# One-hot products of the routing in bf16, two of them on GpSimd, and a gate exponential issued earlier

## The chip, the cores and the metric

The kernel runs on one core of one Trainium2 chip. The metric is the device time of one execution in microseconds. A core has a matrix engine (TensorE, PE in the profile; PEld is its weight load), a vector engine (VectorE, DVE), an activation engine (ScalarE, ACT), GpSimd (POOL) and a queue that issues most DMAs (SyncE, SP). The engines run side by side and wait for each other only through semaphores; each engine takes its own instructions in order.

## The reference

Three parts follow one another: attention over 4 x 8 heads of 576 tokens, a gated feed-forward with a spatial mix, and a mixture of 8 experts. The change is in the routing of the third part. In short:

```python
logits = einsum('bsd,de->bse', x, w_gate)              # 4 x 576 tokens, 8 experts
local_gate = 1 / (1 + exp(-(x @ w_local)))
for b, s in tokens:                                    # in order within a batch row
    fresh = argmax(logits[b, s])
    e = fresh if s == 0 or local_gate[b, s] < 0.5 else prev_e
    p = softmax(logits[b, s])
    out[b, s] = p[e] * (relu(x[b, s] @ w1[e]) @ w2[e])
```

So every token gets one expert, which may be the one of the token before it, and a weight p[e].

## The kernel before

The kernel is written engine by engine, with the order of each engine set by hand and with semaphores between them; no planner is at work. Tokens lie as 128 partitions by F = 20 columns (5 tiles of 128 rows by 4 batch rows, the last tile partly filled). After the last feed-forward group the routing works out, for each token, a position in a list sorted by expert. The list is cut into NSLOT = 25 tiles of 128 rows, each tile of one expert. A token's position is then a tile number (`tile_of`) and a row number (`row_of`).

The table `slots` (128 rows by 25 tiles by 2 numbers: the token number and the weight) is made by products on TensorE. VectorE makes `tile_hot` (L1274: 1 where the column is the token's tile, 20 x 25 numbers on each partition), `entries` (L1277 and L1279: `tile_hot` times the token number, kept as the number less 2304 in `token_less`, and `tile_hot` times `weight`) and `row_hot` (L1283: 1 where the column is the token's row, in five parts of 4 x 128 numbers). All are f32. As each part of `row_hot` is ready, TensorE takes 4 products `row_hot` x `entries` (L1343) into one bank, 20 products in all, each adding 50 columns. VectorE reads the sums out of the bank into `slots` (L1295 and L1296).

The helper `step` is what sets the pace of VectorE here: it gives an instruction an increment of the semaphore `routed`, and lets VectorE wait for that same increment before it goes on. `mark` keeps the count under a name for other engines to wait for.

The order on VectorE around this stretch is: last small steps on positions, `tile_hot`, `weight` (L1276, without a wait of its own), two `entries`, five parts of `row_hot`, three copies of the steering numbers (L1287, L1290), then `low_parts(dve, (0, 0, 1), "w1")`, which makes the low halves of the first expert's w1 in four pieces (L1120), and only then the wait for `slots_summed` and the two copies into `slots`. After that come the low halves of w2, again four pieces. Each piece of L1120 waits for its high half, a cast of ScalarE (L1476), and that waits until the expert's weights have landed.

When `slots` is there, GpSimd copies the token numbers of a tile (L1396) and gathers the 128 token rows by an indirect DMA (L1399). TensorE turns them (L1596), ScalarE and VectorE split them into a high and a low part (L1481, L1536), and the expert products begin (L1611 to L1613). From there TensorE runs through all tiles to the end.

Ahead of the routing, in the last group of tokens, ScalarE copies five turned tiles of x2 from the two places of `tbank` to SBUF (L912); each is stored to DRAM by SP, in two DMAs (L864 after the fourth tile, L867 after the fifth), and SP's loads of the expert weights (L1358, L1360) wait until both stores have landed. TensorE may turn tile m only when tile m-2 has been copied (a wait on `x2_out`). The logits are turned after the second tile and taken to SBUF by VectorE (L996). After its five copies ScalarE loads another activation table and takes the two exponentials, of the gate (L1303) and of the logits less their maximum (L1305), and VectorE waits for both ahead of L1215.

Of the kernel before, what the change touches and what calls it, by code (L numbers as in the profile page):

```python
# [5 lines left out]
ALU = mybir.AluOpType  # L6
ACT = mybir.ActivationFunctionType
# [10 lines left out]
def moe_block(nc, q, k, v, s, w_in, g_ln, w_sg, b_sg, w_out, w_gate, w_local, w1, w2, out):  # L18
# [34 lines left out]
    with stack:  # L53
# [31 lines left out]
        iota_p = sb("iota_p", [P, P], F32)  # L85
        token_less = sb("token_less", [P, ST, B], F32)
# [109 lines left out]
        tile_of = eb("tile_of", [P, F], F32)  # L196
        row_of = eb("row_of", [P, F], F32)
        tile_hot = eb("tile_hot", [P, F, NSLOT], F32)
        entries = eb("entries", [P, F, 2, NSLOT], F32)
        row_hot = eb("row_hot", [P, F, P], F32)  # L200
# [98 lines left out]
        slots_summed = sem("slots_summed")  # L299
        expert_in = [sem(f"expert_in{e}") for e in range(E)]  # L300
# [535 lines left out]
        CONSTS = 6 + 9  # L836
# [37 lines left out]
        def _(act):  # L874
# [27 lines left out]
            def tokens_out(b):  # L902

                for n in range(2):
                    act.wait_ge(logits_mm, 2 * b + n + 1)
                    nc.scalar.copy(logT[:, halves[n]], obank[0:E + 1, n, 0:HALF]).then_inc(logT_done, 1)
                act.wait_ge(x2_stored, 16 * (FROM + 2 * b))
                stand_alone(act)
                for m in range(ST):
                    r = rows_of[m]  # L910
                    act.wait_ge(x2_turned, ST * b + m + 1)
                    nc.scalar.copy(x2[0:r, m, :], tbank[0:r, m % 2, :]).then_inc(x2_out, 1)  # L912

# [10 lines left out]
            tokens_out(B - 1)  # L924
# [212 lines left out]
        def _(pool):  # L1137
# [41 lines left out]
            nc.gpsimd.iota(token_less[:, :, :], pattern=[[P, ST], [S, B]], base=-TOK, channel_multiplier=1,  # L1179
# [3 lines left out]
        def _(dve):  # L1183
# [87 lines left out]
            def over_tokens(x, n):  # L1271
# [3 lines left out]
                                         over_tokens(iota_t[:, :], NSLOT), ALU.is_equal))  # L1275
            nc.vector.tensor_reduce(weight[:, :, :], weigh[:, :, :, :], AX_X, ALU.add)  # L1276
            step(nc.vector.tensor_tensor(entries[:, :, 0, :], tile_hot[:, :, :],  # L1277
                                         over_columns(token_less[:, :, :].rearrange("p t b -> p (t b)"), NSLOT), ALU.mult))
            step(nc.vector.tensor_tensor(entries[:, :, 1, :], tile_hot[:, :, :],  # L1279
                                         over_columns(weight[:, :, :].rearrange("p t b -> p (t b)"), NSLOT), ALU.mult))  # L1280
# [14 lines left out]
            step(nc.vector.tensor_scalar(slots[:, :, 0].bitcast(I32), obank[:, 1, 0:NSLOT], float(TOK), None, ALU.add))  # L1295
            step(nc.vector.tensor_copy(slots[:, :, 1], obank[:, 1, NSLOT:2 * NSLOT]))  # L1296
            mark("slots_done")

        @block.scalar
        def _(act):  # L1300
            lg = logit[:, :, :, :].rearrange("p b t e -> p (b t) e")
            act.wait_ge(logits_left, FROM + B)
            nc.scalar.activation(rgate[:, :], lg[:, :, E], ACT.Exp, scale=-1.0).then_inc(route_exp, 1)  # L1303
            act.wait_ge(routed, 2)
            nc.scalar.activation(rexp[:, :, :], rdiff[:, :, :], ACT.Exp).then_inc(route_exp, 1)  # L1305

        @block.tensor
        def _(pe):
# [31 lines left out]
            for n in range(ST):  # L1340
                pe.wait_ge(routed, marks[f"rows_done{n}"])
                for f in range(n * B, (n + 1) * B):
                    mm = nc.tensor.matmul(obank[:, 1, 0:2 * NSLOT], row_hot[:, f, :],  # L1343
                                          entries[:, f, :, :].rearrange("p a n -> p (a n)"),
                                          start=(f == 0), stop=(f == F - 1))
# [39 lines left out]
        def _(pool):  # L1385
            pool.wait_ge(x2_stored, 16 * (FROM + 2 * B))
            pool.wait_ge(zero_stored, 16)
            pool.wait_ge(routed, marks["slots_done"])
# [344 lines left out]
```

## Time and profile before

| | us |
|---|---|
| median of 3 runs | 942.02 |
| lowest and highest | 939.26, 942.26 |
| span of the profiled execution | 940.1 |
| PE busy in it | 873.8 (93%) |
| DVE busy | 517.7 (55%) |
| ACT busy | 405.3 (43%) |
| POOL busy | 99.3 (11%) |

The profile is of one execution. Its page gives busy times, the chain of work that ended last, and the costliest groups of instructions; the timeline gives single instructions with their start, and the idle time of the engine before them with what ended it. L12 is line 12 of the kernel. The granted clock of TensorE is 1.00 at 2.4 GHz and 0.50 at 1.2 GHz.

### The profile page before, as it was taken

Reading aid. Unit: us, or ns where it says so; the run is one execution under the profiler, and the core shown is the slowest. Engines: PE = TensorE matmul, PEld = TensorE weight load, DVE = VectorE, ACT = ScalarE, POOL = GpSimd, SP = SyncE. Lnnn points to the kernel's source line nnn. Section 1 sums busy time; section 2 is a strip of 40 time slices with the busy share of each in tenths; the row PEclk is TensorE's granted clock in tenths of the full one; section 3 lists DMA queues with packets and bytes.
Section 4 is the critical chain, followed back from the end, with each engine's and each line's share of the span. In section 5 each row is a group of like instructions: output and inputs, shape, how many; then the busy total and the mean of one; then the engine's idle time right before and its main releaser. Section 6 shows DMA issues by size and latency. Waiting matters only on the chain.

```text
span 940.1 us, 19053 instructions
## 1 busy us (share of the span) xinstructions
PE 873.8 (93%) x5573; PEld 725.9 (77%) x5574; DVE 517.7 (55%) x1021; ACT 405.3 (43%) x990; POOL 99.3 (11%) x187
## 2 busy tenths in 40 slices
PE   4899999999999989999999999748999999999993
PEld 2677778787787769988988989546888888888773
DVE  6567767777677743624535335384556266536221
ACT  2566666666666644215134142233435244415110
POOL 0001111111111020000000000001111111111111
PEclk9999999999999989999999999858999999999997
DMA  6422232222323100001001001196345255511100
GB/s 165 146 66 66 58 70 53 67 62 58 71 52 71 39 20 1 1 1 50 0 0 50 0 0 52 57 351 224 117 147 201 77 199 205 210 49 35 38 33 21
DMA packets 100842, 74.88 MB, mean 80 GB/s; under 512 B 81416, under 2 KB 81416, under 8 KB 100778
## 3 DMA queue, kind: packets, MB, share of 16 engines
q1 hardware_dynamic: 96810, 63.21, 22.1%
q0 software_dynamic: 4000, 11.28, 3.7%
q8 instruction: 16, 0.26, 0.1%
q14 instruction: 16, 0.13, 0.0%
HBM read 64.43 MB, written 11.86 MB: 81 GB/s over the span
## 4 chain that ended last, share of the span: by engine, by line
PE 90%; DVE 3%; DMA 2%; SPq 2%; issue 2%; ACT 1%; POOL 0%; POOLq 0%; ACTq 0%; DVEq 0%
PE sbank L1020 24%; PE obank L728 10%; PE sbank L1611 9%; PE sbank L1613 9%; PE sbank L1612 9%; PE tbank L709 5%; PE sbank L694 5%; PE sbank L696 3%; PE obank L719 2%; PE tbank L672 2%; PE obank L1068 2%; PE tbank L677 1%; PE tbank L1596 1%; PE tbank L1636 1%; PE sbank L701 1%
## 5 line engine op out<-in xcount | busy, mean ns | idle before, releaser
L455 ACT ACTIVATE probs<-sbank,nmax 128x128 f32<-128x128 f32 (+4 forms) x160 | 90.8, 568 | 55.3 <-DVE nmax L585 55.2
L728 PE MATMUL obank<-pT,v_raw 128*64 128x128 f32 (+2 forms) x960 | 113.2, 262 | 0.3 <-ACT recipT L474 0.3
L728 PEld LDWEIGHTS obank<-pT,v_raw 128*64 128x64 f32 (+1 forms) x960 | 91.5, 136 | 11.4 <-ACT recipT L474 0.5
L585 DVE TENSOR_REDUCE nmax<-sbank 128x1 f32<-128x128 f32 (+4 forms) x160 | 86.5, 541 | 15.4 <-PE sbank L701 12.0
L694 PE MATMUL sbank<-k,q 128*128 128x256 f32 (+2 forms) x192 | 76.6, 404 | 0.8 <-ACT probs L455 0.8
L1611 PE MATMUL sbank<-w_high,xsT_h 128*128 x184 | 74.8, 407 | 2.0 <-DVE xsT_l L1536 1.7
L1120 DVE TENSOR_TENSOR w_low<-w_low,w_high (+1 forms) x64 | 74.0, 1216 | 0.7 <-ACT w_high L1476 0.3
L709 PE MATMUL tbank<-ident,probs 128*128 128x128 f32 (+2 forms) x480 | 73.9, 267 | 0.2 <-ACT probs L455 0.2
L1613 PE MATMUL sbank<-w_low,xsT_h 128*128 x184 | 72.6, 395 | 0.0
L1612 PE MATMUL sbank<-w_high,xsT_l 128*128 x184 | 72.4, 394 | 0.0
L1611 PE MATMUL sbank<-w_high,hidT_h 128*128 x176 | 70.9, 403 | 0.2
L1476 ACT CAST w_high<-w_low (+1 forms) x64 | 62.3, 1052 | 17.4 <-SPq L1365 17.4
L1613 PE MATMUL sbank<-w_low,hidT_h 128*128 x176 | 68.8, 391 | 0.0
L1612 PE MATMUL sbank<-w_high,hidT_l 128*128 x176 | 68.6, 390 | 0.0
L696 PE MATMUL sbank<-k,q 128*128 128x256 f32 (+2 forms) x192 | 60.8, 321 | 0.0
L709 PEld LDWEIGHTS tbank<-ident,probs 128*128 128x128 f32 (+2 forms) x480 | 47.6, 139 | 8.3 <-issue 5.6
L1499 ACT CAST hidT_h<-tbank 128x512 fp32r<-128x512 f32 x22 | 12.9, 586 | 92.3 <-PE tbank L1636 92.3
L1572 DVE TENSOR_SCALAR y<-sbank,sid 128x512 f32<-128x512 f32 x22 | 16.5, 750 | 63.6 <-PE sbank L1613 62.7
L591 DVE COPY pT<-tbank 128x256 f32<-128x256 f32 x64 | 35.7, 558 | 26.1 <-PE tbank L709 26.1
L562 DVE TENSOR_TENSOR k<-tbank,k 64x512 fp32r<-64x512 f32 x64 | 28.7, 449 | 38.5 <-ACT q L450 38.2
L1020 PE MATMUL sbank<-wsg_h,vn_h 128*128 128x288 f32 x160 | 47.5, 297 | 2.2 <-DVE vn_l L954 1.9
L1407 POOL DMA_INDIRECT out_dram<-y,sid x25 | 25.3, 1010 | 217.2 <-DVE y L1572 214.1
(230 smaller groups left out, 1983.5 us busy)
## 6 DMA issues: line engine op xcount, KB each, us to landing
w_low<-in_moe_w_dram SPq DMA_DIRECT2D x16, 2048.0 KB, 13.4
k_raw<-in_k_dram SPq DMA_DIRECT2D x64, 128.0 KB, 2.3
q_raw<-in_q_dram SPq DMA_DIRECT2D x32, 128.0 KB, 2.3
v_raw<-in_v_dram SPq DMA_DIRECT2D x32, 128.0 KB, 2.2
x_dram<-x SPq DMA_DIRECT2D x4, 1024.0 KB, 4.4
win_raw<-in_moe_w_in_dram SPq DMA_DIRECT2D x1, 2048.0 KB, 8.0
wsg_raw<-in_moe_w_sg_dram SPq DMA_DIRECT2D x1, 1152.0 KB, 6.3
k_raw<-in_k_dram SPq DMA_DIRECT2D x64, 16.0 KB, 2.1
```

The lines of the kernel that those rows point to most:

```text
L455: nc.scalar.activation(probs_view(u, i, r), score_view(i, r), ACT.Exp, bias=nmax[u][0:r, i:i + 1], accum_out=sums[u][0:r, i:i + 1]).then_i ...
L585: nc.vector.tensor_reduce(nmax[u][0:r, i:i + 1], src, ax, ALU.max, negate=True).then_inc(maxed, 1)
L694: nc.tensor.matmul(dst, q1[u][:, q_cols], k1[u][:, cols], start=True, stop=False)
L696: nc.tensor.matmul(dst, q2[u][:, q_cols], k2[u][:, cols], start=False, stop=last)
L709: mm = nc.tensor.transpose(tbank[0:c, 1 if i == 3 else 0, r * j:r * (j + 1)], probs[u][0:r, OFF_P[i] + P * j:OFF_P[i] + P * j + c], ident[ ...
L728: mm = nc.tensor.matmul(obank[0:D, c, a:a + w], v_raw[u][0:r, j, :], pT[0:r, j, P * i:P * i + w], start=(j == 0), stop=(j == i))
L1020: mm = nc.tensor.matmul(dst, a[:, i, lhs_cols], b[:, i, rhs_cols], start=(n == 0), stop=(n == 3 * len(pairs) - 1))
L1120: nc.vector.tensor_sub(w, w.bitcast(F32), piece(w_high, high_place, i).bitcast(F32)).then_inc(wlow_done, 1)
L1476: nc.scalar.copy(piece(w_high, high_place, i), piece(w_low, low_place, i).bitcast(F32)).then_inc(whigh_done, 1)
L1611: nc.tensor.matmul(dst, xh, wh, start=first, stop=False)
L1612: nc.tensor.matmul(dst, xl, wh, start=False, stop=False)
L1613: return nc.tensor.matmul(dst, xh, wl, start=False, stop=last)
```

## The change

The numbers of the one-hot products become bf16. So that nothing is lost, the token number is split in two parts that bf16 holds exactly (a multiple of 64 in `token_high`, 0 to 127 in `token_low`), and the weight in three (`weight_parts`), each being the bf16 rounding of what is left. `entries` so has 5 parts of 25 columns in place of 2. The two of the token number are made by GpSimd, the three of the weight by VectorE. The sums of the parts are taken after the products. The exponential of the gate, with the table load ahead of it, is issued between the second and the third copy of the last group.

```diff
-        iota_p = sb("iota_p", [P, P], F32)
-        token_less = sb("token_less", [P, ST, B], F32)
+        iota_p = sb("iota_p", [P, P], BF16)
+        slot_ids = sb("slot_ids", [P, NSLOT], F32)
+        iota_tb = sb("iota_tb", [P, NSLOT], BF16)
+        token_low = sb("token_low", [P, ST, B], BF16)
+        token_high = sb("token_high", [P, ST, B], BF16)
...
-        tile_of = eb("tile_of", [P, F], F32)
-        row_of = eb("row_of", [P, F], F32)
-        tile_hot = eb("tile_hot", [P, F, NSLOT], F32)
-        entries = eb("entries", [P, F, 2, NSLOT], F32)
-        row_hot = eb("row_hot", [P, F, P], F32)
+        tile_of = eb("tile_of", [P, F], BF16)
+        row_of = eb("row_of", [P, F], BF16)
+        tile_hot = eb("tile_hot", [P, F, NSLOT], BF16)
+        entries = eb("entries", [P, F, 5, NSLOT], BF16)
+        row_hot = eb("row_hot", [P, F, P], BF16)
+        weight_parts = [eb(f"weight_part{n}", [P, ST, B], BF16) for n in range(3)]
+        weight_left = [eb(f"weight_left{n}", [P, ST, B], F32) for n in range(2)]
...
+            def gate_exps():
+                act.wait_ge(logits_left, FROM + B)
+                nc.scalar.activation(rgate[:, :], logit[:, :, :, E].rearrange("p b t -> p (b t)"), ACT.Exp,
+                                     scale=-1.0).then_inc(route_exp, 1)
...
                     nc.scalar.copy(x2[0:r, m, :], tbank[0:r, m % 2, :]).then_inc(x2_out, 1)
+                    if last and m == 1:
+                        gate_exps()
...
             step(nc.vector.tensor_tensor(tile_hot[:, :, :], over_columns(tile_of[:, :], NSLOT),
-                                         over_tokens(iota_t[:, :], NSLOT), ALU.is_equal))
-            nc.vector.tensor_reduce(weight[:, :, :], weigh[:, :, :, :], AX_X, ALU.add)
-            step(nc.vector.tensor_tensor(entries[:, :, 0, :], tile_hot[:, :, :],
-                                         over_columns(token_less[:, :, :].rearrange("p t b -> p (t b)"), NSLOT), ALU.mult))
-            step(nc.vector.tensor_tensor(entries[:, :, 1, :], tile_hot[:, :, :],
-                                         over_columns(weight[:, :, :].rearrange("p t b -> p (t b)"), NSLOT), ALU.mult))
+                                         over_tokens(iota_tb[:, :], NSLOT), ALU.is_equal))
+            mark("tiles_hot")
+            step(nc.vector.tensor_reduce(weight[:, :, :], weigh[:, :, :, :], AX_X, ALU.add))
+            step(nc.vector.tensor_copy(weight_parts[0][:, :, :], weight[:, :, :]))
+            step(nc.vector.tensor_tensor(weight_left[0][:, :, :], weight[:, :, :], weight_parts[0][:, :, :],
+                                         ALU.subtract))
+            step(nc.vector.tensor_copy(weight_parts[1][:, :, :], weight_left[0][:, :, :]))
+            step(nc.vector.tensor_tensor(weight_left[1][:, :, :], weight_left[0][:, :, :],
+                                         weight_parts[1][:, :, :], ALU.subtract))
+            step(nc.vector.tensor_copy(weight_parts[2][:, :, :], weight_left[1][:, :, :]))
+            for n in range(3):
+                step(nc.vector.tensor_tensor(entries[:, :, 2 + n, :], tile_hot[:, :, :],
+                                             over_columns(weight_parts[n][:, :, :].rearrange("p t b -> p (t b)"),
+                                                          NSLOT), ALU.mult))
...
-            step(nc.vector.tensor_scalar(slots[:, :, 0].bitcast(I32), obank[:, 1, 0:NSLOT], float(TOK), None, ALU.add))
-            step(nc.vector.tensor_copy(slots[:, :, 1], obank[:, 1, NSLOT:2 * NSLOT]))
+            parts = obank[:, 1, 0:5 * NSLOT].rearrange("p (a n) -> p n a", n=NSLOT)
+            step(nc.vector.tensor_reduce(slot_ids[:, :], parts[:, :, 0:2], AX_X, ALU.add))
+            step(nc.vector.tensor_scalar(slots[:, :, 0].bitcast(I32), slot_ids[:, :], float(TOK), None, ALU.add))
+            step(nc.vector.tensor_reduce(slots[:, :, 1], parts[:, :, 2:5], AX_X, ALU.add))
...
-                    mm = nc.tensor.matmul(obank[:, 1, 0:2 * NSLOT], row_hot[:, f, :],
+                    if f == 0:
+                        pe.wait_ge(tokens_in, 2)
+                    mm = nc.tensor.matmul(obank[:, 1, 0:5 * NSLOT], row_hot[:, f, :],
...
             pool.wait_ge(zero_stored, 16)
+            pool.wait_ge(routed, marks["tiles_hot"])
+            for n, t in enumerate((token_high, token_low)):
+                x = t[:, :, :].rearrange("p t b -> p (t b)").rearrange("p (f o) -> p f o", o=1)
+                nc.gpsimd.tensor_tensor(entries[:, :, n, :], tile_hot[:, :, :],
+                                        x.broadcast_to([P, F, NSLOT]), ALU.mult).then_inc(tokens_in, 1)
```

Left out above: three small `iota` instructions of GpSimd in place of one, among its constants, and the two lines that took the gate's exponential at its old place.

## Rows read from the trace of the kernel before

**Rows 1.** The page, part 4: the chain that ended last, by engine.

```profile
PE 90%; DVE 3%; DMA 2%; SPq 2%; issue 2%; ACT 1%; POOL 0%; POOLq 0%; ACTq 0%; DVEq 0%
```

**Rows 2.** Windows: from:to, length, PE, PEld, DVE, ACT, POOL busy, clock, DMA, GB/s.

```profile
628.00:631.00 3.00, 3.00 (x15) 2.89 (x14) 2.53 (x3) 2.56 (x3) 0.00 (x0) 0.50 1.05 388
...
639.00:640.00 1.00, 0.74 (x2) 0.65 (x3) 0.01 (x1) 0.00 (x0) 0.74 (x1) 0.50 0.00 0
...
643.00:644.00 1.00, 1.00 (x5) 0.79 (x4) 0.00 (x0) 0.00 (x0) 0.00 (x0) 0.82 1.04 426
```

**Rows 3.** Timeline, one-hot stretch: start, length, engine, line, tiles, shapes, count [idle before].

```profile
619.18 0.67 DVE L1274 TENSOR_TENSOR tile_hot<-tile_of,iota_t 128x500 f32<-128x500 f32 x1
619.89 0.32 DVE L1276 TENSOR_REDUCE weight<-weigh 128x20 f32<-128x160 f32 x1
620.12 0.67 DVE L1277 TENSOR_TENSOR entries<-tile_hot,token_less 128x500 f32<-128x500 f32 x1
620.83 0.68 DVE L1279 TENSOR_TENSOR entries<-tile_hot,weight 128x500 f32<-128x500 f32 x1
...
622.29 8.77 PE L1343 MATMUL obank<-entries,row_hot 128*128 128x50 f32 x40 [4.07 <-DVE row_hot L1283]
...
625.90 4.63 DVE L1120 TENSOR_TENSOR w_low<-w_low,w_high 128x1024 fp32r<-128x1024 f32 x4
631.09 0.18 DVE L1295 TENSOR_SCALAR slots<-obank 128x25 int32<-128x25 f32 x1 [0.56 <-PE obank L1343]
631.31 0.18 DVE L1296 COPY slots<-obank 128x25 f32<-128x25 f32 x1
...
631.74 4.63 DVE L1120 TENSOR_TENSOR w_low<-w_low,w_high 128x1024 fp32r<-128x1024 f32 x4 [0.24 <-DVE slots L1296]
```

**Rows 4.** Timeline, the last token copies, the exponentials and the first steps behind them.

```profile
601.23 0.20 DVE L996 COPY logit<-obank 128x45 f32<-128x45 f32 x1 [5.57 <-PE obank L1087]
...
602.54 0.60 PE L1077 MATMUL tbank<-ident,x2T 128*64 128x128 f32 x4 [0.33 <-ACT x L912]
...
603.18 0.58 ACT L912 COPY x<-tbank 64x512 f32<-64x512 f32 x1 [0.29 <-PE tbank L1077]
603.77 1.28 ACT L1303 ACT_TABLE_LOAD   x1
...
605.21 0.32 ACT L1305 ACTIVATE rexp<-rdiff 128x160 f32<-128x160 f32 x1
605.63 0.18 DVE L1215 TENSOR_SCALAR rgate<-rgate 128x20 f32<-128x20 f32 x1 [2.14 <-ACT rexp L1305]
605.85 0.28 DVE L1216 RECIPROCAL rkeep<-rgate 128x20 f32<-128x20 f32 x1
```

**Rows 5.** Timeline, SP's first weight load and ScalarE's casts of the weights.

```profile
608.97 0.40 SPq L1358 DMA_DIRECT2D w_low<-in_moe_w_dram  x1
...
622.89 7.67 ACT L1476 CAST w_high<-w_low 128x1024 fp32r<-128x1024 f32 x8 [17.36 <-SPq L1365]
```

**Rows 6.** Groups by line and shape, 598 to 640 us: busy us, mean ns, idle before.

```profile
L1283 DVE TENSOR_TENSOR row_hot<-row_of,iota_p 128x512 f32<-128x512 f32 x5 | 3.5, 691 | 0.2
...
L1206 DVE TENSOR_TENSOR rdiff<-logit,rmax 128x160 f32<-128x160 f32 x1 | 0.3, 324 | 0.0
...
L1207 DVE TENSOR_SCALAR requal<-rdiff 128x160 f32<-128x160 f32 x1 | 0.2, 243 | 0.0
```

**Rows 7.** POOL: two groups by line and shape of the whole span, then single instructions.

```profile
L427 POOL CAST q<-q 64x576 fp32r<-64x576 f32 x32 | 21.1, 661 | 175.2 <-ACT q L450 175.2
L432 POOL COPY recip_wide<-recip 128x320 f32<-128x320 f32 x32 | 14.4, 449 | 124.4 <-DVE recip L605 124.4
...
631.67 0.19 POOL L1396 COPY gid<-slots 128x1 int32<-128x1 int32 x1 [285.49 <-DVE slots L1296]
...
634.02 1.27 POOL L1396 COPY gid<-slots 128x1 int32<-128x1 int32 x1
```

**Rows 8.** Timeline, 636 to 640 us: where TensorE starts again.

```profile
636.49 1.12 PE L1596 MATMUL tbank<-ident,xs 128*128 128x128 f32 x4 [5.43 <-DMA xs<-x_dram,gid]
...
639.26 0.79 PE L1611 MATMUL sbank<-w_high,xsT_h 128*128 x1 [1.66 <-DVE xsT_l L1536]
```

More of the change, by code:

```diff
@@ L299, in moe_block @@
         slots_summed = sem("slots_summed")
+        tokens_in = sem("tokens_in")
         expert_in = [sem(f"expert_in{e}") for e in range(E)]
@@ L831, in _ @@
             slot(HEADS + 1, 1, this=False, before=False, after=False)
-        CONSTS = 6 + 9
+        CONSTS = 6 + 11
         MIX, PROJ, VEE, YOU = 0, 2 * KT, 4 * KT, 4 * KT + ST
@@ L900, in gated_high, with tokens_out @@
                     nc.scalar.copy(g_h[:, n % KT, halves[n // KT]], uT[:, n % KT, halves[n // KT]]).then_inc(gh_done, 1)
-            def tokens_out(b):
+            def gate_exps():
+                act.wait_ge(logits_left, FROM + B)
+                nc.scalar.activation(rgate[:, :], logit[:, :, :, E].rearrange("p b t -> p (b t)"), ACT.Exp,
+                                     scale=-1.0).then_inc(route_exp, 1)
+            def tokens_out(b, last=False):
                 for n in range(2):
@@ L923, in _ @@
             gated_high(B - 1)
-            tokens_out(B - 1)
+            tokens_out(B - 1, last=True)
         @block.vector
@@ L1178, in _ @@
                            allow_small_or_imprecise_dtypes=True).then_inc(route_const, 1)
-            nc.gpsimd.iota(token_less[:, :, :], pattern=[[P, ST], [S, B]], base=-TOK, channel_multiplier=1,
+            nc.gpsimd.iota(iota_tb[:, :], pattern=[[1, NSLOT]], base=0, channel_multiplier=0,
+                           allow_small_or_imprecise_dtypes=True).then_inc(route_const, 1)
+            nc.gpsimd.iota(token_high[:, :, :], pattern=[[P, ST], [S, B]], base=-TOK, channel_multiplier=0,
+                           allow_small_or_imprecise_dtypes=True).then_inc(route_const, 1)
+            nc.gpsimd.iota(token_low[:, :, :], pattern=[[0, ST], [0, B]], base=0, channel_multiplier=1,
                            allow_small_or_imprecise_dtypes=True).then_inc(route_const, 1)
@@ L1301, in _ @@
             lg = logit[:, :, :, :].rearrange("p b t e -> p (b t) e")
-            act.wait_ge(logits_left, FROM + B)
-            nc.scalar.activation(rgate[:, :], lg[:, :, E], ACT.Exp, scale=-1.0).then_inc(route_exp, 1)
             act.wait_ge(routed, 2)
```

## The prediction

> **What bounds the kernel now.** I read the page's chain first: TensorE holds 90% of it and VectorE 3% [rows 1]. The routing is the place where that is not so. The windows show the granted clock at 0.50 while TensorE takes the one-hot products and still at 0.50 when it starts again at 639.26; only at 643 does it rise [rows 2, 8]. Behind it TensorE runs tile after tile, so what moves the end is the moment at which `slots` is complete: 631.49 us (631.31 + 0.18) [rows 3]. GpSimd waits for it and starts 0.18 us later [rows 7]; the gather, turning and splitting lead to the first expert product at 639.26 [rows 8]. I take that stretch as rigid: what `slots` gains or loses, the end gains or loses.
>
> Next I read the timeline to see which engine makes `slots` late. Two chains meet in it. TensorE's 40 records of L1343 run from 622.29 to 631.06. VectorE meanwhile has done the one-hot work, the steering copies and four pieces of w1's low half, 625.90 to 630.53, and waits 0.56 us for TensorE at L1295 [rows 3]. This is the most important number here: VectorE's own line is only 0.56 us shorter than TensorE's. The pieces of w1 stand ahead of the wait in the program. Whatever is saved on TensorE beyond 0.56 us is not seen.
>
> **TensorE's products.** 40 records become 20, since bf16 needs one pass where f32 shows two records for each product. At 8.77/40 = 0.22 us each that is 4.4 us; the columns rise from 50 to 125, so the bounds are 4.4 and, were nothing saved, 8.77. The first part of `row_hot` is ready at 622.23 + 3.2 = 625.4 by the sum below, and VectorE asks for the sums at 633.8: at the upper bound TensorE would be 0.4 late; at the lower, which I take because the record count halves for certain, the products follow `row_hot` part by part and end over 4 us before VectorE asks. Gain: the 0.56 us, no more.
>
> **VectorE's line, step by step.**
> - The sum over `weigh` now has a wait: 0.32 + 0.04 in place of the 0.23 from 619.89 to 620.12: +0.13 [rows 3].
> - Five small steps, three roundings and two subtractions on 20 numbers, each with a wait: one such step is 605.63 to 605.85, 0.22 us [rows 4]; 5 x 0.22 = +1.10.
> - `entries` for the weight: three products in place of two for both; GpSimd has the others. One takes 0.71 from start to start [rows 3]: +0.71.
> - The nine large instructions (tile_hot, three entries, five row_hot) in bf16: no 2-byte VectorE instruction is in the trace. Bounds: unchanged (0.67 and 0.69), or half the time per element. The time per element is (669 - 324)/(500 - 160) = 1.01 ns for two inputs; half of it saves 0.25 on each of four and 0.26 on each of five, 2.3 in all. An instruction with one input does show a faster rate at the same size (243 against 324 ns for 160 numbers) [rows 3, 6]. I take unchanged: every large two-input row has 1.0 ns per element, and the repeated operand does not get denser by being narrower.
> - The sums out of the bank: before 0.40 (631.09 to 631.49). After: a reduction of 50 numbers, a scalar step, a reduction of 75. From 0.32 for 160 at 1.01 ns less per number, 0.21 and 0.24; with two waits of 0.04 and the 0.18, 0.71: +0.31 [rows 3, 6].
>
> The unchanged rate has a rule of the Trainium skill behind it, which speaks against this change: the page Vector Engine (DVE) Microarchitecture Reference, section 5.1, says that a two-input instruction takes two 16-bit elements per cycle only if the innermost step of every operand is 1 or -1, and that one element read again and again as an operand ran at one per cycle. Here each of the nine has such an operand. No run here shows it yet; by it the 2.3 us stay unsaved.
>
> **The gate's exponential.** Today the last copy ends at 603.76, then come the table load of 1.28, the gate and `rexp`, which ends at 605.53; VectorE has waited 2.14 for it [rows 4]. Moved, the table load begins once the logits are in SBUF (601.43), ends near 602.75, and the gate near 603.0. The third and fourth copies follow, each 0.54, to 604.1. The fifth tile can only be turned when the third copy is done (603.55) and takes 0.60, so its copy runs 604.2 to 604.8 [rows 4], and `rexp` ends at about 605.12. Gain 0.41. Bounds: 0, and 0.64, the two waits of ScalarE that the load can fill. The price: the two stores of x2, and SP's queue of weight loads behind them, move by the delay of the fourth and fifth copies, about 1.0 us. The load issued at 608.97 goes out near 609.9, and the casts begin at 623.9 in place of 622.89 [rows 5]. VectorE wants the first cast, done at 624.9, at 627.4 or later (625.90 + 1.5) [rows 3]; it is covered by 2.5 us, and by 0.2 even if the 2.3 us above were saved. Without that cover it would cost up to 1.0.
>
> **GpSimd beside VectorE.** The trace has no two-input GpSimd instruction. One input costs (661 - 449)/(576 - 320) = 0.83 ns a number and 0.18 fixed, so 500 numbers are 0.60 us; read one input after the other, 1.01 [rows 7]. TensorE's new wait `tokens_in` is harmless: even at 1.01 each both are done before 622.5, ahead of the first part of `row_hot`. What matters is a row that looks small: GpSimd's copy at 634.02 takes 1.27 us where the same copy took 0.19, and it lies across VectorE's two-input pieces of w1, 1.16 each from 631.74, ending as the third of them ends [rows 3, 7]. So one of the two was kept out of SBUF while the other's instruction ran. The reverse, VectorE kept waiting by GpSimd, is not in the trace. Bounds: 0, and 2 x 1.01 = 2.02. I take an exclusive turn for both, as that row shows. GpSimd starts 0.18 after tile_hot, at 620.03, to 621.04; VectorE's sum has one input and passes, its first rounding would start at 620.25 and waits 0.79; the second product holds the subtraction or the rounding 0.9 more: +1.7, behind which all of VectorE's line is queued, the w1 pieces and `slots` with it.
>
> The rule of the Trainium skill beside it (SBUF — State Buffer, Who interferes with whom) is that VectorE instructions with two SBUF inputs, or in a two-port mode, and GpSimd instructions that read SBUF exclude each other for a whole instruction, whichever began first. The row at 634.02 agrees in one direction. GPSIMD Engine Reference, section 3.1, prices a two-input instruction at 4497 ns for 2048 numbers; an estimate from it is 1.2 us for 500, by which the sum would be about 0.4 us larger.
>
> **The sum.** VectorE's arrival at `slots`: 0.13 + 1.10 + 0.71 - 0.41 + 1.7 = +3.23. Less the 0.56 it no longer waits, with 0.04 between instructions, plus 0.31: `slots` is 3.0 us later, 634.5. Against the profiled execution that is a span of 940.1 + 3.0 = 943.1. The median of the runs is 1.9 above that span, and the shift is carried over to it: 942.02 + 3.0 = 945.0.
>
> **The rivals.**
> 1. No exclusion, rate unchanged. The same sum without 1.7: +1.3, 943.3. For it: the trace shows only GpSimd waiting, so VectorE may have the right of way. Against: an instruction of GpSimd already under way can hardly be stopped.
> 2. Faster, the other side: the nine instructions run at half the time per element, -2.3, and VectorE is not held. Sum 1.3 - 2.3 = -1.0, 941.0. It decides from the point where the nine save more than 1.3 us together, 0.15 each. For it: narrower numbers, and the faster one-input row [rows 6]. Against: the repeated operand. With the exclusion as well it gives +0.7, 942.7.
> 3. GpSimd's products take twice as long, 2.0 us each, for a reason the rows don't show, and hold VectorE throughout: 2 us more, 947.0. `tokens_in` itself would decide only from about 5 us each.
> 4. The change does little, since its target was TensorE's 8.77 us: that is part of each case, the 0.56.
>
> TensorE's clock adds a spread to all: it rose 4.0 us after the restart at 639.26 [rows 2, 8]; each us of that more or less is 0.5 us of products at 1.2 in place of 2.4 GHz. The three runs before span 939.26 to 942.26.
>
> **How the numbers follow.** Forecast 0.55 (945.0, own range 943.8 to 946.5); rival 1 0.23; rival 2 0.14, half of it with the exclusion; rival 3 0.08. The range from 941.5 to 947.0 leaves the faster half of rival 2 and the upper tail outside. A measurement of this kernel tells 0.3% from no change, 2.8 us. Slower by more: two thirds of the forecast and nearly all of rival 3, 0.43. Within: the other third, rivals 1 and 2, 0.53. Faster: 0.04, only rival 2 with a kind clock.
>
> **What would show it.** In the new profile: the nine instructions at 0.67 to 0.69 us (or 0.4: rival 2); a VectorE step of 20 numbers near 620.3 that takes 0.8 to 1 us in place of 0.18 (or none: rival 1); GpSimd's two rows at 1.0 us; no wait at the first read of the bank; L1343's successor with 20 records, done 4 us before VectorE comes; the table load at 601.5. The prediction is wrong if `slots` is not later, or if the stretch from `slots` to 639.26 is not rigid.

## The result and the profile after

| | before | after |
|---|---|---|
| median of 9 runs, us | 941.17 | 944.42 |
| lowest and highest | 939.26, 942.26 | 942.43, 946.05 |
| span of the profiled execution | 940.1 | 944.3 |
| TensorE's part of the chain | 90% | 90% |

The changed kernel is slower: ratio 1.0038, 95% interval 1.0028 to 1.0049. The forecast was 945.0, 3.0 us above the kernel before; measured are 3.25 us.

The profiled execution of the changed kernel is the slowest of its nine (946.05). The two profiled executions differ by 4.2 us, of which 1.16 arose ahead of the change: VectorE's last copy of the logits out of the bank starts at 601.23 before [rows 4] and at 602.39 after. So from here on moments are counted from the start of that copy, and written "at +12.3". Ahead of it the change touches only a few small constants of GpSimd, and in the other profiles below the copy starts between 598.38 and 601.51, so this part moves from execution to execution. What is left of the 4.2 is 3.04.

The timeline of the changed kernel, from `tile_hot` to the second part of the weights (start, length, engine, line, operation, tiles, shapes, idle time before and what ended it):

```profile
619.91 0.67 DVE L1291 TENSOR_TENSOR tile_hot<-tile_of,iota_tb 128x500 bf16<-128x500 bf16 x1
620.61 0.32 DVE L1294 TENSOR_REDUCE weight<-weigh 128x20 f32<-128x160 f32 x1
620.76 1.02 POOL L1418 TENSOR_TENSOR entries<-tile_hot,token_high 128x500 bf16<-128x500 bf16 x1 [273.16 <-DVE tile_hot L1291]
620.97 0.85 DVE L1295 CAST weight_part<-weight 128x20 bf16<-128x20 f32 x1
621.74 1.03 POOL L1418 TENSOR_TENSOR entries<-tile_hot,token_low 128x500 bf16<-128x500 bf16 x1
621.85 0.95 DVE L1296 TENSOR_TENSOR weight_left<-weight,weight_part 128x20 f32<-128x20 f32 x1
622.83 0.18 DVE L1298 CAST weight_part<-weight_left 128x20 bf16<-128x20 f32 x1
...
623.47 2.11 DVE L1303 TENSOR_TENSOR entries<-tile_hot,weight_part 128x500 bf16<-128x500 bf16 x3
...
625.61 3.60 DVE L1308 TENSOR_TENSOR row_hot<-row_of,iota_p 128x512 bf16<-128x512 bf16 x5
626.36 3.51 PE L1370 MATMUL obank<-entries,row_hot 128*128 128x125 bf16 x20 [7.41 <-DVE row_hot L1308]
...
629.98 4.63 DVE L1133 TENSOR_TENSOR w_low<-w_low,w_high 128x1024 fp32r<-128x1024 f32 x4
634.52 0.20 DVE L1321 TENSOR_REDUCE slot_ids<-obank 128x25 f32<-128x50 f32 x1
634.76 0.18 DVE L1322 TENSOR_SCALAR slots<-slot_ids 128x25 int32<-128x25 f32 x1
634.98 0.24 DVE L1323 TENSOR_REDUCE slots<-obank 128x25 f32<-128x75 f32 x1
```

The reader is to see four things beside [rows 3]. TensorE's products are done at 629.87, 40 records in 8.77 us having become 20 in 3.51, and VectorE asks for the sums only at 634.52, with no idle time left in front of that row. The large instructions have kept their 0.67 to 0.69 each (`row_hot`: 3.60 from the start of the first to the end of the fifth, 3.59 before). Two small steps on 20 numbers, L1295 and L1296, take 0.85 and 0.95 where their like take 0.18, and each ends 0.03 or 0.04 after a product of GpSimd. And `slots` is complete at +32.83 (634.98 + 0.24 - 602.39), against +30.26 before.

The copies and exponentials, to be set beside [rows 4]:

```profile
602.64 1.28 ACT L910 ACT_TABLE_LOAD   x1
603.93 0.24 ACT L910 ACTIVATE rgate<-logit 128x20 f32<-128x20 f32 x1
...
605.42 0.58 ACT L923 COPY x<-tbank 64x512 f32<-64x512 f32 x1 [0.29 <-PE tbank L1090]
605.91 0.34 ACT L1330 ACTIVATE rexp<-rdiff 128x160 f32<-128x160 f32 x1
...
606.35 0.18 DVE L1232 TENSOR_SCALAR rgate<-rgate 128x20 f32<-128x20 f32 x1 [1.69 <-ACT rexp L1330]
...
611.46 0.40 SPq L1385 DMA_DIRECT2D w_low<-in_moe_w_dram  x1
```

VectorE goes on at +3.96 in place of +4.40; the weight load goes out at +9.07 in place of +7.74 [rows 5].

### The profile page after: what moved, and what is told of

Same layout as the page of the kernel before. It is cut to its first block, busy times and chain, and to the rows that moved or that the text cites. A ratio compares the mean times of both kernels' runs of the same rounds, so it can differ in the third digit from the quotient of the medians.

```text
span 944.3 us, 19025 instructions
## 1 busy us (share of the span) xinstructions
PE 870.0 (92%) x5553; PEld 720.4 (76%) x5554; DVE 521.2 (55%) x1028; ACT 405.3 (43%) x990; POOL 102.0 (11%) x191
## 4 chain that ended last, share of the span: by engine, by line
PE 90%; DVE 4%; issue 2%; DMA 1%; ACT 1%; SPq 1%; POOL 0%; POOLq 0%; ACTq 0%; DVEq 0%
PE sbank L1033 24%; PE obank L734 11%; PE sbank L1643 9%; PE sbank L1645 9%; PE sbank L1644 9%; PE tbank L715 6%; PE sbank L700 5%; PE sbank L702 3%; PE obank L725 2%; PE tbank L678 2%; PE obank L1081 2%; PE tbank L683 2%; PE sbank L707 1%; PE tbank L1628 1%; PE tbank L1668 1%
```

## The experiments

The moments of all profiles, in us from the start of the last copy of the logits:

| kernel | tile_hot | slots complete | first expert product | median us |
|---|---|---|---|---|
| before | 17.95 | 30.26 | 38.03 | 941.0 to 941.3 |
| changed | 17.52 | 32.83 | 40.64 | 944.42 |
| e1, gate alone | 17.51 | 29.83 | 37.61 | 939.94 (one run) |
| e2, no GpSimd | 17.51 | 32.80 | 40.61 | 944.31 |
| e3, before with slots first | 17.96 | 30.34 | 39.06 | 942.08 |
| e4, changed with slots first | 17.50 | 28.27 | 37.00 | 940.01 |
| e5, three products | 17.51 | 33.53 | 41.28 | 944.80 (one run) |
| e6, write only | 17.51 | 32.00 | not comparable | not comparable |
| e7, innermost step 1 | 17.51 | 30.59 | 38.45 | 942.32 |
| e9, e4 with the copy ahead | 17.51 | 28.27 | 37.08 | 939.17 |
| e10, all together | 17.51 | 27.60 | 36.78 | 940.14 |
| e11, e9 with the load held | 17.50 | 28.28 | 36.16 | 939.54 |
| e12, entries at step 1, load held | 17.50 | 27.81 | 35.73 | 939.32 |

**One part alone (e1).** The edit: the kernel before with the gate's exponential at its new place (`gate_exps` as in the change).

```diff
+                    if last and m == 1:
+                        gate_exps()
...
-            act.wait_ge(logits_left, FROM + B)
-            nc.scalar.activation(rgate[:, :], lg[:, :, E], ACT.Exp, scale=-1.0).then_inc(route_exp, 1)
```

> One part alone: the kernel before with nothing changed but the gate's exponential, issued between the second and the third copy of the last group. Moments are counted from the start of VectorE's last copy of the logits out of the bank, since the part of the program ahead of it moves by about 1 us from execution to execution. In the kernel before, tile_hot begins at 17.95 and slots is complete at 30.26. My theory: the table load fills waits of ScalarE, tile_hot begins 0.4 earlier (17.5), but slots is complete only 0.4 earlier too (29.8), because TensorE's 8.8 us of products start behind row_hot; the weight load goes out 1.3 later (9.1 in place of 7.7). Rival: the later stores and loads of the weights hold the w1 pieces (first piece in place of 24.7 not before 24.3 + 1), and slots gains nothing or loses up to 1.

`slots` is complete 0.43 earlier, as is `tile_hot` (0.44). The load goes out at +8.30, 0.56 later than before and not 1.3: how late it goes differs between profiles with the same copies ahead of it (+8.24 in e4, +9.07 in the changed kernel). The rival falls: VectorE begins the w1 pieces at +24.23, 0.44 earlier than before, and waits for no cast. Two rows of e1's timeline:

```profile
623.68 4.63 DVE L1127 TENSOR_TENSOR w_low<-w_low,w_high 128x1024 fp32r<-128x1024 f32 x4
628.88 0.18 DVE L1302 TENSOR_SCALAR slots<-obank 128x25 int32<-128x25 f32 x1 [0.56 <-PE obank L1348]
```

The wait of 0.56 for TensorE is still there. So this part of the change is worth its 0.4 us at `slots`, and the rest of the change costs 3.0 there: +32.83 against +29.83. The single time of 939.94 does not show the 0.4: in this execution the copy of the logits itself came 1.78 earlier than before (599.45 against 601.23).

**The token products back on VectorE (e2).**

```diff
-            for n, t in enumerate((token_high, token_low)):          # GpSimd
-                nc.gpsimd.tensor_tensor(entries[:, :, n, :], tile_hot[:, :, :], ...).then_inc(tokens_in, 1)
+            for n, t in enumerate((token_high, token_low)):          # VectorE
+                step(nc.vector.tensor_tensor(entries[:, :, n, :], tile_hot[:, :, :], ..., ALU.mult))
```

> The changed kernel with the two token-number products on VectorE again, in bf16, in place of GpSimd, and TensorE's wait for GpSimd gone. Same counting; in the changed kernel slots is complete at 32.83. My theory (VectorE and GpSimd exclude each other while both want SBUF): the first rounding falls from 0.85 to 0.18 us and the first subtraction from 0.95 to 0.18, and two more products of 0.71 take the place of these 1.4, so slots is complete within 0.2 of 32.8 and the time is that of the changed kernel, some 944.4. Rival (the 0.85 and 0.95 belong to the rounding to bf16 and the subtraction themselves): they stay, and slots is complete near 34.2, some 1.4 us slower.

VectorE's small steps in the timeline of e2:

```profile
620.08 0.17 DVE L1295 CAST weight_part<-weight 128x20 bf16<-128x20 f32 x1
620.29 0.18 DVE L1296 TENSOR_TENSOR weight_left<-weight,weight_part 128x20 f32<-128x20 f32 x1
...
621.13 0.68 DVE L1303 TENSOR_TENSOR entries<-tile_hot,token_high 128x500 bf16<-128x500 bf16 x1
```

Both long steps are short again and `slots` is complete at +32.80, the same as with GpSimd; the ratio to the kernel before is 1.0035 (1.0022 to 1.0048). Handing two products of 0.71 each to an idle engine saved 1.42 us of VectorE's work and cost it 1.44 of waiting (0.85 + 0.95 - 2 x 0.18).

**A third product (e5).**

```diff
-            for n, t in enumerate((token_high, token_low)):
+            for n, t in enumerate((token_high, token_low, token_low)):
...
+                pool.wait_ge(tokens_in, n)
-                nc.gpsimd.tensor_tensor(entries[:, :, n, :], ...)
+                nc.gpsimd.tensor_tensor(entries[:, :, min(n, 1), :], ...)
...
-                        pe.wait_ge(tokens_in, 2)
+                        pe.wait_ge(tokens_in, 3)
```

> The changed kernel with a third product on GpSimd (the second one taken once more into the same place), each waiting for the one ahead of it: the suspected cost by one more. The result is the same. Same counting; tile_hot begins at 17.5. My theory (each GpSimd product keeps VectorE out of SBUF while it reads): the third one holds the second rounding or the second subtraction, 0.18 in the changed kernel, to some 0.9, and slots is complete at 33.6 in place of 32.83. Rival (VectorE has to wait only where both want to start together, at the first two): slots stays at 32.8 and all later steps at 0.18.

GpSimd's products and VectorE's small steps in the timeline of e5:

```profile
619.03 1.03 POOL L1419 TENSOR_TENSOR entries<-tile_hot,token_high 128x500 bf16<-128x500 bf16 x1 [273.45 <-DVE tile_hot L1291]
619.18 0.91 DVE L1295 CAST weight_part<-weight 128x20 bf16<-128x20 f32 x1
620.12 0.18 DVE L1296 TENSOR_TENSOR weight_left<-weight,weight_part 128x20 f32<-128x20 f32 x1
620.13 2.20 POOL L1419 TENSOR_TENSOR entries<-tile_hot,token_low 128x500 bf16<-128x500 bf16 x2
620.33 0.89 DVE L1298 CAST weight_part<-weight_left 128x20 bf16<-128x20 f32 x1
621.26 0.18 DVE L1299 TENSOR_TENSOR weight_left<-weight_left,weight_part 128x20 f32<-128x20 f32 x1
621.47 0.89 DVE L1301 CAST weight_part<-weight_left 128x20 bf16<-128x20 f32 x1
```

Three products, three held steps of 0.9, and `slots` at +33.53, 0.70 later. The subtractions that fall between two products of GpSimd pass at 0.18. The theory holds and the rival falls: the cost goes with the number of products. Here the held steps are all roundings, with one input; in the changed kernel one is the subtraction L1296, with two.

**Writing without reading (e6).** The kernel leaves the token numbers out: both places are set to zero, every slot names the spare row, and nothing is stored; only the stretch up to `slots` can be compared.

```diff
-            for n, t in enumerate((token_high, token_low)):
...
-                nc.gpsimd.tensor_tensor(entries[:, :, n, :], tile_hot[:, :, :], ...).then_inc(tokens_in, 1)
+            for n in range(2):
+                nc.gpsimd.memset(entries[:, :, n, :], 0.0).then_inc(tokens_in, 1)
```

> The changed kernel with GpSimd's two products replaced by two memsets of the same places: they write the same 500 bf16 numbers on each partition and read nothing. It leaves the token numbers out: every slot then names the spare row, so the gathers read that row and nothing is stored; only the stretch up to slots is comparable. My theory (it is GpSimd's reading that excludes VectorE's second input): the first subtraction is back at 0.18, and slots is complete near 31.4, 1.4 earlier than in the changed kernel. The first rounding has one input and could use both ports, so it may still wait 0.2 to 0.4. Rival (any GpSimd work on SBUF excludes VectorE): both wait, by the memset's 0.4 to 0.6 each, slots at 32.0 to 32.4.

The same place in the timeline of e6:

```profile
616.71 1.01 POOL L1417 MEMSET entries<- 128x500 bf16 x2 [273.28 <-DVE tile_hot L1291]
616.95 0.80 DVE L1295 CAST weight_part<-weight 128x20 bf16<-128x20 f32 x1
617.78 0.18 DVE L1296 TENSOR_TENSOR weight_left<-weight,weight_part 128x20 f32<-128x20 f32 x1
```

The first rounding is held 0.62, until both memsets are over, so here GpSimd held a one-input VectorE step while it only wrote. The subtraction begins after them (617.78, the memsets end at 617.72) and says nothing, although its 0.18 is what my theory asked for. `slots` came at +32.00, not at my 31.4 but at the lower end of the rival's range. That it is the reading that excludes VectorE's two-input instructions is not shown; what is shown is that GpSimd need not read to hold a rounding.

**The order on VectorE (e3, e4).** Both kernels take the sums before the w1 pieces, and the first low part of x before the w2 pieces.

```diff
-            low_parts(dve, (0, 0, 1), "w1")
             dve.wait_ge(slots_summed, 1)
...
             mark("slots_done")
+            low_parts(dve, (0, 0, 1), "w1")
...
-            low_parts(dve, (0, 0, 1), "w2")
             dve.sem_inc(y_out, FROM)
             x_low(0)
+            low_parts(dve, (0, 0, 1), "w2")
```

> The kernel before with one change of order on VectorE: the wait for slots_summed and the copies into slots come ahead of the four w1 pieces, and the first low part of x comes ahead of the four w2 pieces. My theory: TensorE's products end at the same moment, so VectorE waits some 5 us for them and slots gains nothing (30.2 to 30.3); the first expert product stays at 38.0 to 38.1 and the time within 0.5 us of the kernel before. Rival (the place of the w1 pieces costs by itself, even with f32 products): slots earlier by up to 0.5, or the first expert product later because the pieces now lie between the gather and it.

> The changed kernel with that same change of order. My theory: TensorE's products, now short, end with row_hot at about 27.4, VectorE takes the sums at 27.6, and slots is complete at 28.3 in place of 32.83, 4.5 us earlier than in the changed kernel and 2.0 earlier than in the kernel before. The time would be about 944.4 - 4.5 = 940.0, 0.2% below the kernel before. Rival: the gather now moves its rows while expert 1's weights are still landing (they end at 32.5 in the changed kernel) and takes longer than 3.7 us, which gives back up to 2 us: time up to 942. Second rival: the w1 pieces, ended near 33.0, hold x's low part: no more than 0.5.

With f32 products `slots` gains nothing (+30.34): VectorE waits 5.30 for TensorE. With bf16 products the same edit brings it from +32.83 to +28.27, the 4.5 forecast. So the w1 pieces hid what was saved on TensorE beyond the first 0.56. The ratios to the kernel before are 1.0004 (0.9992 to 1.0015) for e3 and 0.9986 (0.9977 to 0.9995) for e4. The median of e4 is 940.01, that of the changed kernel 944.42, and 944.31 in e2, whose runs were taken together with those of e4.

In both I had missed something, and that e4's 940.0 came out as forecast is partly luck: the medians lie 4.3 apart, but the first products only 3.6. In e3 the first expert product came 1.0 later than before, not at the same moment, and in e4 it came 3.6 earlier than in the changed kernel, although `slots` had gained 4.6. The first two of these four rows of e4's timeline show why; the last two are for the comparison with e9 below:

```profile
629.40 4.65 DVE L1133 TENSOR_TENSOR w_low<-w_low,w_high 128x1024 fp32r<-128x1024 f32 x4
629.43 1.24 POOL L1428 COPY gid<-slots 128x1 int32<-128x1 int32 x1 [7.97 <-DVE slots L1322]
...
631.66 1.19 POOL L1431 DMA_INDIRECT xs<-x_dram,gid  x1 [0.99 <-POOL gid L1428]
...
635.33 1.12 PE L1628 MATMUL tbank<-ident,xs 128*128 128x128 f32 x4 [6.76 <-DMA xs<-x_dram,gid]
```

GpSimd's copy of the token numbers, 0.19 before [rows 7], takes 1.24: VectorE's first w1 piece now begins 0.03 ahead of it, where before the first w2 piece began 0.07 behind it (631.74 against 631.67 [rows 3, 7]). In e3 it takes 1.14 for the same reason. It is the same exclusion, the other way round; e9 tries it.

**No repeated operand (e7).** The tables are laid out with the token column innermost and the counting tables stored in full; the nine large instructions then have innermost step 1 everywhere.

```diff
-        tile_hot = eb("tile_hot", [P, F, NSLOT], BF16)
-        entries = eb("entries", [P, F, 5, NSLOT], BF16)
-        row_hot = eb("row_hot", [P, F, P], BF16)
+        tile_hot = eb("tile_hot", [P, NSLOT, F], BF16)
+        entries = eb("entries", [P, 5, NSLOT, F], BF16)
+        row_hot = eb("row_hot", [P, ST, P, B], BF16)
```

> The changed kernel with the one-hot tables laid out the other way: the token columns innermost, and the counting tables stored in full, so that no operand of the nine large VectorE instructions repeats one element; all are bf16 with innermost step 1. GpSimd's products read and write the new layout too, and TensorE reads its weights with a step of 4 elements and its columns with a step of 20. My theory (the repeated operand, not bf16 as such, kept the nine at 0.67 to 0.70): they fall to about 0.41 and 0.42, 2.3 us in all, and slots is complete at 30.5 in place of 32.83; time near 942. Rival (two inputs never go faster here): 0.67 stays and slots at 32.8, time 944.4. Second rival: the stepped reads slow TensorE, its 20 products take more than 0.4 each and end later than VectorE asks (30.0): slots later by that.

The large instructions and TensorE's products in the timeline of e7:

```profile
617.41 0.41 DVE L1288 TENSOR_TENSOR tile_hot<-tile_of,iota_tb 128x500 bf16<-128x500 bf16 x1
...
620.84 1.33 DVE L1300 TENSOR_TENSOR entries<-tile_hot,weight_part 128x500 bf16<-128x500 bf16 x3
622.21 2.26 DVE L1305 TENSOR_TENSOR row_hot<-row_of,iota_p 128x512 bf16<-128x512 bf16 x5
622.69 4.67 PE L1367 MATMUL obank<-entries,row_hot 128*128 128x125 bf16 x20 [6.24 <-DVE row_hot L1305]
```

0.67 became 0.41, and five parts of `row_hot` take 2.26 in place of 3.60. `slots` is complete at +30.59 (30.5 expected); ratio to the kernel before 1.0012 (1.0000 to 1.0023). The layout without bf16 would hardly have done it: the w1 pieces, f32 with two inputs and no repeated operand, take 4.63 for four of 1024 numbers, 1.13 ns a number [rows 3], where e7 has 0.41 us for 500. The rate is a matter of the operand's step, as the Trainium skill has it (Vector Engine (DVE) Microarchitecture Reference, section 5.1), and not of two inputs as such.

**The copy ahead of the pieces (e9).** e4 with one wait more.

```diff
             mark("slots_done")
+            dve.wait_ge(gid_done, 1)
             low_parts(dve, (0, 0, 1), "w1")
```

> The changed kernel with slots ahead of the w1 pieces, as before, and one more wait: VectorE begins the first w1 piece only when GpSimd has made its first copy of the token numbers. With the order alone slots was complete at 28.27 but GpSimd's copy took 1.24 in place of 0.19, behind the first w1 piece, and the first expert product began at 37.00 (38.03 in the kernel before, 40.64 in the changed one). My theory: the copy is back at 0.19 and everything behind it comes 1.05 earlier, first product at 35.95, time 1 us below that of the order alone, near 939. Rival (gather and weight load of expert 1, which ends near 32, share the DMA engines now): the gather takes over 3.8 us and the gain is less than 0.5.

The copy, the gather and the turning of its rows in the timeline of e9:

```profile
628.73 0.19 POOL L1429 COPY gid<-slots 128x1 int32<-128x1 int32 x1 [7.96 <-DVE slots L1322]
629.00 4.63 DVE L1133 TENSOR_TENSOR w_low<-w_low,w_high 128x1024 fp32r<-128x1024 f32 x4 [0.34 <-POOL gid L1429]
629.90 1.38 POOL L1432 DMA_INDIRECT xs<-x_dram,gid  x1 [0.99 <-POOL gid L1429]
...
634.70 1.11 PE L1629 MATMUL tbank<-ident,xs 128*128 128x128 f32 x4 [6.84 <-DMA xs<-x_dram,gid]
```

The copy is 0.19 again, so the theory of the exclusion holds for it, and the gather goes out 1.05 earlier, at +29.51. But TensorE turns its rows at +34.31, 4.80 later in place of 3.67 in e4. The first product stayed, at +37.08: the forecast of 35.95 fell, the rival held. Time 939.17, ratio 0.9980 (0.9968 to 0.9993): near the 939 forecast, but by luck, since the first product came no earlier than in e4 and the two intervals overlap. In this profile the load of the weights had also gone out 0.79 later than in e4 (+9.03 against +8.24); the next run, with +9.02, is without that difference.

**The load of expert 1 held back (e11).**

```diff
             load(0)
-            load(1)
+            load_half(1, 0)
             relay(0)
+            sp.wait_ge(routed, marks["slots_done"])
+            sp.wait_ge(gathered[0], 16)
+            load_half(1, 1)
+            sp.wait_ge(gathered[1], 16)
             relay(1)
-            sp.wait_ge(routed, marks["slots_done"])
-            for u in range(2):
-                sp.wait_ge(gathered[u], 16)
             load(2)
```

> The kernel of the run in which the first copy is ahead of the w1 pieces, with one change of SP's order: the w2 half of expert 1's weights is loaded only after the first gather has landed, in place of before it. There, the gather was issued 1.05 earlier than with the order alone and landed no earlier, while the load of expert 1 ran until 33.3. My theory (gather and load share the DMA engines): the gather, issued at 29.5, is back at 3.6 to 3.7 from issue to TensorE's turning (33.2 in place of 34.31), the first expert product comes at 36.0 in place of 37.08, time near 938.5. Rival (the gather's length comes from VectorE and GpSimd in SBUF, its descriptors being written beside the w1 pieces): it still takes 4.8 and the first product stays at 37.1. Second rival: the held half is late for expert 1 (its casts begin near 48) and costs time later; it should land by 40.

The gather and the turning in the timeline of e11:

```profile
630.25 1.38 POOL L1442 DMA_INDIRECT xs<-x_dram,gid  x1 [0.99 <-POOL gid L1439]
...
634.12 1.12 PE L1639 MATMUL tbank<-ident,xs 128*128 128x128 f32 x4 [5.92 <-DMA xs<-x_dram,gid]
```

From issue to turning it is 3.87, and the first product comes at +36.16, 0.92 earlier than in e9. So the load beside it made up the longer gather: with no load left under way the same stretch took 3.64 before and 3.80 in the changed kernel. The median, 939.54 (0.9984; 0.9974 to 0.9995), is no better than that of e9: the moment at which the clock rises, below, takes half of the gain back, and the measurement does not resolve the rest.

**All together (e10, e12).** e10 is e9 with the tables of e7 and all products on VectorE; e12 is the same with `row_hot` in its first layout and the load held.

> All together: the new layout with innermost step 1, all five products for the entries on VectorE, slots ahead of the w1 pieces, and the first w1 piece behind GpSimd's first copy. My theory: from tile_hot at 17.5, 0.45 + 0.36 + 1.05 + 5 x 0.45 + 5 x 0.45 + 0.74, then the sums: slots complete at about 25.4, against 30.26 in the kernel before; gather and turning as ever put the first expert product at 33.2; time near 936.5. Rival: the weight loads set the pace. The casts of w1 begin near 22.6 and its low pieces end by 30.5, which is early enough, but the gather then runs wholly beside the load of expert 1 (to about 32) and may take 2 us more: first product at 35, time near 938. Second rival: TensorE's stepped reads take longer than VectorE's parts (0.45) and end the gain at 20 x their length.

> The run before it, with tile_hot and entries laid out with innermost step 1 and all five products on VectorE, but row_hot as in the changed kernel, so that TensorE reads its weights without a step (its columns with a step of 20). My theory: 17.5 + 0.45 + 0.36 + 1.05 + 5 x 0.45 + 3.6 + 0.74: slots complete at 26.7 in place of 28.3, TensorE not waited for, as its 20 products follow row_hot at 0.18 each; gather issued at 28.0, turning at 31.7, first expert product at 34.5, time near 937. Rival: the step of 20 in the columns is what slowed TensorE to 0.233 a product when both had steps; then its 4.7 us end near 26.5 and slots comes at 27.2. Second rival: the first half of expert 1's load (to about 28) still meets the gather, or ScalarE's casts of expert 0, which end at 31, hold x's high part: first product no earlier than 35.

Both missed their first products, by 3.6 and 1.2 us, and mostly for the reason named as a rival. TensorE's 20 products take 4.67 in e10 and 4.62 in e12, and now VectorE waits for them. From the timeline of e10:

```profile
627.21 0.21 DVE L1320 TENSOR_REDUCE slot_ids<-obank 128x25 f32<-128x50 f32 x1 [2.26 <-PE obank L1369]
```

and from that of e12:

```profile
622.65 4.62 PE L1371 MATMUL obank<-entries,row_hot 128*128 128x125 bf16 x20 [5.84 <-DVE row_hot L1308]
...
627.38 0.21 DVE L1322 TENSOR_REDUCE slot_ids<-obank 128x25 f32<-128x50 f32 x1 [1.15 <-PE obank L1371]
```

The weights' step is gone in e12 and the 0.23 a product remained, so it is the step of 20 in the columns that costs it (at most 0.18 without, 3.51 for 20 in the changed kernel). In e10 the gather ran wholly beside expert 1's load, 5.06 from issue to turning. e10 measures 0.9989 (0.9977 to 1.0000), e12 0.9976 (0.9966 to 0.9986), 939.32 against 941.08: e12 is faster than the kernel before, by 0.24%, and than the changed one. e9 and e12 can't be told apart.

## Why the prediction was right

**VectorE's line bounds, not TensorE's: right.** The 0.56 was the whole gain of the products, and e3 and e4 show it from both sides. TensorE ended 4.65 before VectorE asked; over 4 was said.

**The terms.** The reduction's wait: 0.36 from start to start, as said. The five small steps: in e2, without GpSimd, 1.05 (620.08 to 621.13) against 1.10. One more product: 3 x 0.71, as said. The rate of the nine: unchanged, as said and for the reason said (e7). The sums out of the bank: 0.70 from start to end, said 0.71; they began 0.1 before the last w1 piece had ended, where the sum had them begin 0.04 behind it: 0.13 of the difference. The gate: 0.43 and 0.41. Its price was put too low: the load went out 1.33 later and the casts began 1.55 later (+23.21 against +21.66), where 1.0 was said. They stayed covered, since VectorE takes up the first w1 piece only at +27.59.

**The exclusion: right in kind, 1.44 in place of 1.7.** It was argued before from one row in the other direction [rows 7]; L1295, L1296 and e2, e5 now show it in this one. The two holds are 0.67 and 0.77, where 0.79 and 0.9 were said: the prediction let a held step take its 0.18 behind the end of GpSimd's product, while the rows show it ended 0.03 or 0.04 behind it. The 1.01 for one product was right to 0.02; that its two inputs are read one after the other was not tried apart. One reading was wrong without harm to the sum: the pieces from 631.74 [rows 3], beside which the copy at 634.02 waits, are those of w2, not of w1.

**The rival of no exclusion** had its price nearly right: take the 1.44 away from the 2.57 on `slots` and 1.1 us would be left, where 1.3 was said. e2 is not that case, since the products have to be made somewhere. **The faster rival** was right in its 2.3 (2.24 from the changed kernel to e7), but not for this change: it takes e7's layout. With the exclusion that stands at +0.33 on `slots`, where +0.7 was said.

**The rigid stretch: nearly.** `slots` moved by 2.57 and the first product by 2.61. But the clock did not move along. Two windows of the changed kernel (columns as in [rows 2]), to be set beside [rows 2]:

```profile
647.00:648.00 1.00, 1.00 (x4) 0.77 (x3) 0.00 (x0) 0.00 (x0) 0.00 (x0) 0.52 1.03 414
648.00:649.00 1.00, 1.00 (x6) 0.82 (x5) 0.00 (x0) 0.60 (x1) 0.00 (x0) 1.00 1.01 414
```

The granted clock goes from 0.50 to 1.00 just before 648.0 (0.52 is the mean of the first window), 4.9 us after the first product at 643.03; before it rose near 643.4, 4.1 us after 639.26 [rows 2, 8]. 0.8 us more at 1.2 in place of 2.4 GHz is 0.4 us of products. 2.61 + 0.4 is 3.0; the medians differ by 3.25, with an interval of 2.6 to 4.6, and the two profiled executions by 3.04 from the copy on. The forecast shift of 3.0 on `slots` was 0.4 too large, and the clock, whose move was in the prediction only as a spread, gave about that back: part of the closeness is luck.

**The carried-over median.** The prediction added its shift of 3.0 to a median of 942.02 from three runs. The median before of nine runs is 941.17, and with 3.0 it would be 944.2; measured are 944.42. The forecast of 945.0 is 0.6 too high, since its base was 0.85 too high and its shift 0.25 too small.

## What to carry to other kernels

Ask which engine asks for the result, not only which one makes it: here the consumer had 4.6 us of other work queued in front of the read, so that 5.3 us saved on the producer gave 0.56 until that work was moved behind it. Work handed to GpSimd beside a busy VectorE can be paid for in VectorE's waits, here 1.44 for a saving of 1.42: count them before counting the saving. In these kernels bf16 made a two-input VectorE instruction faster only once no operand was repeated innermost (0.67 against 0.41); the layout that did it cost TensorE its dense columns (at least 0.05 a product).

## What had not been expected of the hardware

GpSimd's memset, which reads nothing, held a VectorE rounding of 20 numbers for 0.62 us (e6). A gather that was issued beside a weight load took 4.80 to 5.06 us from issue to use (e9, e10), against 3.64 to 3.87 where the load had ended, was about to end or was held back (before, e4, the changed kernel, e12, e11). TensorE takes 0.23 us a bf16 product of 125 columns at a step of 20 elements at the low clock, against at most 0.18 without the step (e12; the changed kernel, where `row_hot` set the pace).

The granted clock rose between +42.1 and +42.6 in the kernel before, e1, e3, e4, e7, e9, e10 and e11, although the first expert product lay anywhere between +36.2 and +39.1 in these. In the changed kernel, e2 and e5, with first products from +40.6 to +41.3, it rose between +45.6 and +46.3, and in e12 at +39.0. Why it rose at these moments stays open. Two of the windows in which it rose, first e11, counted from 600.74:

```profile
642.00:643.00 1.00, 1.00 (x4) 0.76 (x4) 0.00 (x0) 0.58 (x1) 0.00 (x0) 0.55 1.02 395
```

then e12, counted from 600.27:

```profile
639.00:640.00 1.00, 1.00 (x5) 0.77 (x5) 1.00 (x2) 0.00 (x0) 0.00 (x0) 0.88 0.96 313
```

A first product that comes earlier gains only half of that time as long as the rise stays where it is. The profiled executions bear this out. The estimate below is the move of the first product plus half of the change in the time from it to the rise; beside it stands the measured move of the end, counted from the copy of the logits. All are differences to the kernel before, in us, from one execution each:

| kernel | first product | from it to the rise | estimate | end |
|---|---|---|---|---|
| changed | +2.61 | +0.8 | +3.0 | +3.04 |
| e1 | -0.42 | +0.4 | -0.2 | -0.22 |
| e4 | -1.03 | +1.2 | -0.4 | -0.17 |
| e9 | -0.95 | +1.3 | -0.3 | -0.26 |
| e10 | -1.25 | +1.7 | -0.4 | -0.18 |
| e11 | -1.87 | +1.9 | -0.9 | -0.61 |
| e12 | -2.30 | -0.9 | -2.7 | -2.54 |

The estimate comes within 0.3 or so in each. So e1, e4, e9, e10 and e11 give back half or more of what their first products gained, and e12 keeps its gain because the rise came earlier too. No run changed the moment of the rise alone.
